# A Strassen-like product sum kept in PSUM by a ScalarE copy, and the remainder's operands made on VectorE

## What is computed

```python
# attention part: a gated recurrence over S=768 steps, B=2, H=8 heads, D=40 (run in chunks of 128 tokens)
C = f_stab * C + i_stab * outer(v_t, k_t);  n = f_stab * n + i_stab * k_t
y[:, :, t] = sigmoid(o_gate) * (C @ q_t) / maximum(abs(n . q_t), 1.0)
# mixture-of-experts part on x = y as (1536, 320), 4 experts, hidden width 1024
p = domain_probs / (domain_probs.sum(-1, keepdims=True) + 1e-09)
for e in range(4):
    h = np.maximum(x @ w1[e], 0.0)
    out += p[:, e:e + 1] * (h @ w2[e])
```

## Time and profile before

| | us |
|---|---|
| median of 3 runs (421.38 to 422.93) | 422.16 |
| the profiled execution | 421.93 |
| its span, first to last instruction | 420.2 |
| PE busy in it | 405.5 (97%) |
| DVE, POOL, ACT busy | 276.8, 209.5, 191.4 |
| PE idle before its instructions, put down to DVE's L1181 | 5.0 |

### The profile page before, as it was taken

The page is one execution under the profiler, slowest core; times in us unless marked ns, Lnnn a source line. Parts: engine busy times, 40 slices in busy tenths (PEclk is TensorE's granted clock), DMA queues, the critical chain, the costliest instruction groups (busy, mean ns, idle before and its releaser), DMA issues.

```text
span 420.2 us, 7279 instructions
## 1 busy us (share of the span) xinstructions
PE 405.5 (97%) x2650; PEld 389.8 (93%) x2650; DVE 276.8 (66%) x484; ACT 191.4 (46%) x378; POOL 209.5 (50%) x233
## 2 busy tenths in 40 slices
PE   8999999999999999999996999989999999999997
PEld 8899999998999999999995989877999999999997
DVE  5885796759545448355369862468767776787853
ACT  4575477858352657324033422524443345333420
POOL 4865734577831759604109801653555536456300
PEclk9999999999999999999999899999999999999999
DMA  8899839676860605305034001221122201230002
GB/s 266 271 289 397 350 105 357 217 250 242 278 267 0 222 2 220 123 1 211 0 67 99 0 2 68 97 81 42 41 83 81 81 10 73 83 97 18 1 2 94
DMA packets 18053, 54.49 MB, mean 130 GB/s; under 512 B 2177, under 2 KB 8850, under 8 KB 16866
## 3 DMA queue, kind: packets, MB, share of 16 engines
q1 hardware_dynamic: 17442, 52.63, 36.4%
q10 hardware_dynamic: 576, 1.40, 1.0%
HBM read 50.40 MB, written 2.05 MB: 125 GB/s over the span
## 4 chain that ended last, share of the span: by engine, by line
PE 84%; DVE 8%; issue 3%; POOL 3%; ACT 2%; DVEq 0%; ACTq 0%; POOLq 0%
PE hid_ps L1602 18%; PE acc_ps L1621 18%; PE acc_ps L1685 14%; PE out_ps L1558 4%; PE hid_ps L1685 3%; PE acc_ps L1602 2%; PE out_ps L1565 2%; PE out_ps L1661 2%; PE out_ps L1662 2%; PE out_ps L1664 2%; PE out_ps L1663 2%; PE hid_ps L1451 1%; PE score_ps L1502 1%; PE add_ps L1661 1%; PE score_ps L1661 1%
## 5 line engine op out<-in xcount | busy, mean ns | idle before, releaser
L1181 DVE SCALAR_TENSOR_TENSOR h_lo<-hid_ps,h_hi 128x384 fp32r<-128x384 f32 (+1 forms) x70 | 35.9, 513 | 89.2 <-ACT h_hi L842 88.9
L842 ACT ACTIVATE h_hi<-hid_ps 128x384 fp32r<-128x384 f32 (+1 forms) x70 | 31.9, 456 | 112.4 <-PE hid_ps L1602 112.3
L1621 PE MATMUL acc_ps<-w_hi,h_hi 128*128 128x320 f32 x208 | 66.8, 321 | 6.3 <-DVE h_lo L1181 5.0
L1621 PE MATMUL acc_ps<-w_hi,h_lo 128*128 128x320 f32 x208 | 64.5, 310 | 0.0
L1621 PE MATMUL acc_ps<-w_lo,h_hi 128*128 128x320 f32 x208 | 64.2, 309 | 0.0
L613 POOL TENSOR_TENSOR w_lo<-w_raw,w_hi 128x384 fp32r<-128x384 f32 x40 | 46.8, 1174 | 21.8 <-ACT w_hi L828 21.7
L1602 PE MATMUL hid_ps<-xt_hi,w_hi 128*128 128x384 f32 (+1 forms) x210 | 57.1, 326 | 0.1
L1602 PE MATMUL hid_ps<-xt_hi,w_lo 128*128 128x384 f32 (+1 forms) x210 | 56.6, 323 | 0.0
L1621 PEld LDWEIGHTS acc_ps<-w_hi,h_hi 128*128 128x128 f32 x208 | 39.4, 189 | 8.1 <-DVE h_lo L1181 6.4
L587 POOL TENSOR_SCALAR_AFFINE_SELECT dec_w<-dec_w 128x512 f32<-128x512 f32 x22 | 16.4, 743 | 50.3 <-ACT dec_w L807 50.3
L1621 PEld LDWEIGHTS acc_ps<-w_lo,h_hi 128*128 128x128 f32 x208 | 39.4, 189 | 0.1
(11 more groups left out here) (256 smaller groups left out, 1036.2 us busy)
## 6 DMA issues: line engine op xcount, KB each, us to landing
w_raw<-in_w_b SPq DMA_DIRECT2D x19, 704.0 KB, 7.5
w_raw<-in_w_s SPq DMA_DIRECT2D x12, 832.0 KB, 4.4
raw<-in_qk_s SPq DMA_DIRECT2D x8, 1024.0 KB
g_all<-g_dram SPq DMA_DIRECT2D x10, 512.0 KB, 7.1
kv<-in_kv_n SPq DMA_DIRECT2D x12, 352.0 KB, 6.5
q_pack<-in_q_p SPq DMA_DIRECT2D x10, 192.0 KB, 7.5
out_y<-y_acc SPq DMA_DIRECT2D x12, 160.0 KB, 1.8
carry<-g_dram SPq DMA_DIRECT2D x30, 60.0 KB
```

What stands on the lines that cost most here:

```text
L842: nc.scalar.activation(h_hi[:, M % RING, 0:cols], hid_bank(M)[:, 0:cols], ACT.Relu).then_inc(hid_hi, 1)
L1181: nc.vector.scalar_tensor_tensor(h_lo[:, M % RING, 0:cols], hid_bank(M)[:, 0:cols], 0.0, h_hi[:, M % RING, 0:cols].bitcast(fp32), ALU.max, ...
L1621: last = nc.tensor.matmul(acc_ps[t][:, 0:DM], x, w, start=(f == 0 and i == 0), stop=(f == NF - 1 and i == 2))
```

## The change

Product 1 is copied by ACT from `score_ps` into `out_ps`, and products 6, 7 and 4 accumulate on it; ACT, not DVE, then copies the sums out after product 6 (`keep_2`) and after product 7 (`keep_3`), and `add_21` falls away. The order of the products is 1, 5, 6, 7, 2, 4, 3. One matmul into `out_ps` ahead of step 0 sets that bank up for accumulation. `rest_whole` and `turn_rest` go from POOL to DVE, and the preparation is spread over slots 64 to 74; both `step_sums` on POOL come earlier; step 0's products start in slot 73. Tiles 7 to 11 have their attention, casts and subtractions one slot earlier, with an exception in each table. The loads of the first two weight steps stand in slots 54 and 55 of SP's list.

```diff
-T0 = {2: 2, 3: 6, 4: 16, 5: 22, 6: 30, 7: 35, 8: 41, 9: 47, 10: 51, 11: 57}
+T0 = {2: 2, 3: 6, 4: 16, 5: 22, 6: 30, 7: 34, 8: 40, 9: 46, 10: 50, 11: 56}
-CAST = {4: (11, 12), 5: (16, 17), 6: (24, 25), 7: (28, 31), 8: (36, 38), 9: (42, 44), 10: (45, 48), 11: (52, 53)}
-SUB = {4: (13, 14), 5: (18, 19), 6: (26, 27), 7: (32, 33), 8: (38, 40), 9: (44, 46), 10: (48, 49), 11: (54, 56)}
+CAST = {4: (11, 12), 5: (16, 17), 6: (24, 25), 7: (28, 30), 8: (35, 37), 9: (41, 43), 10: (44, 47), 11: (51, 52)}
+SUB = {4: (13, 14), 5: (18, 19), 6: (26, 27), 7: (31, 32), 8: (37, 39), 9: (43, 45), 10: (47, 48), 11: (53, 55)}
-ORDER = (1, 6, 5, 7, 2, 4, 3)
+ORDER = (1, 5, 6, 7, 2, 4, 3)
-BEGIN = 72
+BEGIN = 73
...
 # SP
-                if M == T0[NT - 1] + 4:
-                    load_step(0)
-                    load_step(1)
+                if M in (54, 55):
+                    load_step(M - 54)
...
 # POOL, slots
-                if M == 64: step_sums(0)
-                if M == 65: own_lows(0); rest_whole(0); turn_rest(1)
-                if M == 66: rest_whole(1); turn_rest(2)
-                if M == 69: step_sums(1)
-                if M == 71: own_lows(1)
+                if M in (59, 61): step_sums((M - 59) // 2)
+                if M in (65, 67): own_lows((M - 65) // 2)
...
 # ACT
-            def keep_1(t):
+            def spread_1(t):
                 act.wait_ge(product_done, product_count(t, 1))
...
-                wait_if(act, whole_of[21], t)
-                nc.scalar.activation(kept_1[:, 0:width(t)], wide_bank[1][:, 0:width(t)], ACT.Copy).then_inc(kept_1_done, 1)
+                wait_if(act, low_of[21], t)
+                nc.scalar.activation(out_ps[:, 0:width(t)], score_ps[:, 0:width(t)], ACT.Copy).then_inc(kept_1_done, 1)
+            def keep_2(t):
+                act.wait_ge(product_done, product_count(t, 6))
+                wait_if(act, whole_of[12], t)
+                nc.scalar.activation(sum_2[:, 0:width(t)], out_ps[:, 0:width(t)], ACT.Copy).then_inc(sum_2_done, 1)
+            def keep_3(t):
+                act.wait_ge(product_done, product_count(t, 7))
+                wait_if(act, whole_of[22], t)
+                nc.scalar.activation(sum_3[:, 0:width(t)], out_ps[:, 0:width(t)], ACT.Copy).then_inc(sum_3_done, 1)
...
 # ACT, slots and steps
-                if M == 79: wide_relu(0, 21); own_highs(2); sums_highs(2)
+                if M == 79: wide_relu(0, 21)
+            own_highs(2)
             wide_relu(0, 12)
+            sums_highs(2)
             wide_relu(0, 22)
             for t in range(1, STEPS):
                 if 1 < t < STEPS - 1:
                     own_highs(t + 1)
-                keep_1(t)
+                spread_1(t)
                 if 1 < t < STEPS - 1:
                     sums_highs(t + 1)
+                keep_5(t)
                 if t + 1 < STEPS:
                     step_down_high(t + 1)
-                keep_5(t)
+                keep_2(t)
+                keep_3(t)
...
 # DVE: add_2, add_3, add_21 removed; slots
+                if M == SLOTS - 1:
+                    add_expert(M // NF, (0,)); wide_low(0, 21); add_expert(M // NF, (1, 2))
+                if M == 64: make_whole(0); turn_whole(0)
+                if M == 65: make_whole(1); turn_whole(1)
+                if M == 66: turn_whole(2); turn_whole(3); sums_lows(0)
+                if M == 67: rest_whole(0); turn_rest(0)
+                if M == 68: rest_whole(1); turn_rest(1)
+                if M == 69: turn_rest(2); turn_rest(3)
+                if M == 70: rest_lows(0)
+                if M == 71: t_lows(0)
+                if M == 72: step_rest_low(0); t_lows(2)
+                if M == 73: rest_lows(1)
+                if M == 74: sums_lows(1); step_rest_low(1)
...
 # PE, in product(t, m)
                 if m == 1:
                     if t == 0:
-                        pe.wait_ge(rest_low, 2)
-                        pe.wait_ge(t_low, 2)
+                        pe.wait_ge(rest_low, 1)
                         pe.wait_ge(p_ready, 2 * NT)
+                        pe.wait_ge(xt_done, NT)
+                        nc.tensor.matmul(out_ps[:, :], left_lo[:, 0, 0, :], xt_hi[:, 0, 0:WIDE], start=True, stop=True)
+                elif m == 5:
+                    pe.wait_ge(sums_low, t + 1)
+                    if t == 0:
+                        pe.wait_ge(rest_low, 2)
+                        pe.wait_ge(t_low, 2)
+                    wait_if(pe, low_of[12], t)
                 elif m == 6:
-                    pe.wait_ge(sums_low, t + 1)
-                    wait_if(pe, low_of[21], t)
+                    pe.wait_ge(kept_1_done, t + 1)
...
-                nc.tensor.matmul(to, hi[:, 0:128], x_hi, start=m in (1, 5, 6), stop=False, skip_group_check=True)
+                nc.tensor.matmul(to, hi[:, 0:128], x_hi, start=m in (1, 5), stop=False, skip_group_check=True)
```

More of the change, by code:

```diff
@@ L743, in _ @@
                     split_low(w)
[L744 to L760, removed]
+                if M in (59, 61):
+                    step_sums((M - 59) // 2)
+                if M in (65, 67):
+                    own_lows((M - 65) // 2)
+                if M in (75, 77):
+                    step_down_low((M - 75) // 2)
+                if M == 78:
                     add_22(0)
-                if M == 78:
                     step_sums(2)
@@ L957, in _ @@
                     gate_open(first)
+                if M == 64:
+                    own_highs(0)
                 if M == 65:
[L959 removed]
                     sums_highs(0)
[L961 to L963 removed]
+                if M == 66:
+                    own_highs(1)
+                    sums_highs(1)
+                if M in (67, 68):
+                    round_t(2 * (M - 67))
                 if M == 69:
                     round_rest(0)
[L966 to L967 removed]
+                if M == 71:
                     round_rest(1)
[L969 to L972 removed]
+                if M == 74:
+                    spread_1(0)
                 if M == 75:
+                    keep_5(0)
                     step_down_high(0)
[L975 removed]
+                if M == 76:
+                    keep_2(0)
                 if M == 77:
+                    keep_3(0)
                     step_down_high(1)
@@ L1183, in hidden_low, with add_expert @@
                     .then_inc(hid_lo, 1)
-            def add_expert(at):
+            def add_expert(at, ts=(0, 1, 2)):
                 load, first_tile, tiles = GROUPS[at]
-                for t in range(tiles):
+                for t in ts[:tiles]:
                     n = first_tile + t
@@ L1358, in _ @@
                     hidden_low(ahead)
-                if M == 79:
-                    wide_low(0, 21)
-                    add_12(0)
                 if M == 0:
@@ L1382, in _ @@
                     keep_heads(k)
-                if M % NF == NF - 1:
+                if M == SLOTS - 1:
+                    add_expert(M // NF, (0,))
+                    wide_low(0, 21)
+                    add_expert(M // NF, (1, 2))
+                elif M % NF == NF - 1:
                     add_expert(M // NF)
@@ L1401, in _ @@
                 if M == 71:
+                    t_lows(0)
+                if M == 72:
+                    step_rest_low(0)
+                    t_lows(2)
+                if M == 73:
                     rest_lows(1)
-                if M == 72:
+                if M == 74:
                     sums_lows(1)
-                if M == 73:
                     step_rest_low(1)
-                if M == 74:
-                    add_2(0)
-                if M == 76:
-                    add_3(0)
                 if M == 78:
                     wide_low(0, 11)
-                    add_21(0)
+            add_12(0)
+            wide_low(0, 12)
             sums_lows(2)
             step_rest_low(2)
-            wide_low(0, 12)
             wide_low(0, 22)
@@ L1425, in _ @@
                 add_wide(t, 2)
-                add_3(t)
                 add_wide(t, 3)
                 wide_low(t, 11)
-                add_21(t)
                 wide_low(t, 21)
```

106 lines of the change are left out of this document (37 added, 69 removed).

## The result

| | before | after |
|---|---|---|
| median, us (4 runs each, side by side) | 422.55 (421.38 to 424.06) | 417.12 (416.24 to 418.35) |
| the profiled execution | 421.93 | 417.27 |
| its span | 420.2 | 415.0 |
| PE, DVE, ACT, POOL busy | 405.5, 276.8, 191.4, 209.5 | 404.0, 243.5, 205.2, 195.5 |

The ratio is 0.987, with a 95% interval of 0.983 to 0.991: the change makes the kernel 1.3% faster. 414.8 had been forecast, with a range of 412.4 to 417.8, so the time is inside the range and 2.3 us above the forecast.

What follows compares the result with a forecast made beforehand. PE was taken as the bound, losing 8.0 us from 219.64 to 247.63 because DVE was late. The terms -8.0 + 0.25 - 1.25 + 1.6 + 0.9 - 0.7 + 0.45 - 0.35 = -7.1 take 421.93 to 414.8, range 412.4 to 417.8.

Steps and rivals of the forecast that it cites:

- rival 1: Slots 64 to 73: DVE stays late, 2 to 4 us of the loss stay, 417 to 419; chance 0.17.
- Part 2: Ahead of product 1 of step 0: one more 512-column matmul on PE's path, +0.25 us.
- Part 3, slots 40 and 56: With the attention tables shifted, PE's waits for evictions at these slots (idle 0.40 each) go, -1.25 us.
- Slot 32: `SUB[7]` puts a subtraction in slot 31 ahead of evictions, delaying PE's first down here: +1.6 us, between 1.2 and 2.2.
- rival 3: Steps: `keep_2` is late in every step by 0.3 to 0.5 us, about 418.5; chance 0.08.
- Part 4: The steps: PE's work unchanged, DVE's freed time worth nothing by itself, only latencies count; +0.3 us in all.
- (a): Steps: `keep_2` delays product 7 by 0.1 us in seven later steps, plus 0.2 once in step 2; +0.9 us.
- (b): Steps 1 and 2: 3.3 us of old waits go, product 5's late operand loses 1.7 and 0.9; -0.7 us.
- (c): Step 11: product 5's operand comes late, as no down follows product 3 of step 10; +0.45 us.
- rival 2: The slot 32 stall does not come and `keep_2` is hidden, 412.5; chance 0.18.
- rival 4: Steps: ACT becomes the bound, product 7 comes 0.8 us later in 11 steps, 423.5, slower than before; chance 0.03.
- rival 5: PE's stalls around 230 us come from semaphores or loads, not DVE's queue; 8.0 us stay, 422.5; chance 0.03.

Runs made afterwards that it cites:

- experiment 5: The kernel of experiment 1 with the remainder's six operations on DVE all in slot 67 instead of 67 to 69; 416.01 us, ratio 0.982.
- experiment 4: The kernel of experiment 1 with the remainder's six operations back on POOL, spread over slots 67 to 69; 415.19 us, ratio 0.980.
- experiment 7: The kernel of experiment 1 with the old product scheme, `keep_1(1)` and `add_2(1)` placed ahead of step 2's preparation; 411.63 us, ratio 0.972.
- experiment 1: The changed kernel with tile 7's two subtractions in slots 32 and 33 instead of 31 and 32; 414.02 us, ratio 0.979.
- experiment 2: The kernel before with tile 7's subtractions moved to slots 31 and 32 and its second cast to slot 30; 425.89 us, ratio 1.007.
- experiment 6: The changed kernel with the old product scheme (SBUF copy, DVE additions, old order, no extra matmul), preparation kept; 419.7 us, ratio 0.992.
- experiment 3: The changed kernel with the tables `T0`, `CAST` and `SUB` as before the change; 415.45 us, ratio 0.983.
- experiment 8: The kernel of experiment 1 with product order 1, 5, 6, 2, 7, 3, 4 in steps 0 to 10 and some downs moved; 411.56 us, ratio 0.971.
- experiment 9: The kernel of experiment 8 with `SUB[10]` at (48, 49) and result 21 ahead of 22 in step 1; 409.86 us, ratio 0.968.

## Why the prediction was right or wrong, step by step

**What bounds the kernel before:** right. The 8.0 us lost in the earlier trace rows came back in full: from M = 65 to 79 the difference moved by 8.7, which is 8.0 less the extra matmul (0.25) and plus the product (0.95) that changed sides. No idle and full clock in 220 to 245 show it, and DVE's operations there have the lengths taken from the earlier trace rows, as in after's

```profile
227.60 1.20 DVE L1257 TENSOR_TENSOR rest_hi<-rest_hi,rest_lo 96x1024 f32<-96x1024 f32 x1
...
244.05 2.28 DVE L1284 TENSOR_TENSOR rest<-rest_lo,rest 32x2048 fp32r<-32x2048 f32 x1
```

The account of DVE's load slot by slot held; rival 1 (DVE stays late) fell. Only its slack had been set a little wide, as the 1.65 us of experiment 5 show, where 1 was expected from it. What the prediction didn't separate was the engine from the place: experiments 4 and 5.

**Part 2, the extra matmul:** +0.25, right: 0.2 by the starts of `hidden_low` in experiment 7, which doesn't have it, against experiment 1.

**Part 3, slots 40 and 56:** right, 0.6 each. **Slot 32: this is the step that failed, by its size.** The prediction named the mechanism, the place and the queue, and gave +1.6, within 1.2 to 2.2, from the subtraction's old place beside POOL. It was 3.3. The idle grew by 2.2, the prediction's upper bound and for its reason, POOL's low part going first (the rows of slot 31 above). At full clock that stall costs 1.9 (experiment 2), inside the bounds; 1.4 came on top at half clock. The sum had left out the clock, though the prediction read in the earlier trace rows that a long idle stood right ahead of half clock there. **The second miss is "behind that slot no other wait is tight":** slot 48 has a wait of 0.33 for the same reason (`SUB[10]` now has a subtraction in slot 47, ahead of the evictions), 0.4 us. The reasoning that worked for slot 31 had not been put to every slot with M = 7 modulo 8. The two misses, 1.7 and 0.4, are the distance between -7.1 and the -5.2 by the spans (0.2 went the other way, ahead of slot 32). So the measured 417.12 lies above the 413.6 to 416.2 that were given to the forecast itself, and inside the stated range only by the part that was kept for rivals 1 and 3, which both fell: the range was right by its width.

**Part 4:** right in its sum (+0.3 predicted, +0.3 measured), but two of its terms are off and cancel, which is luck. (a) Of `keep_2`: 0.1 a step was predicted. In step 3 of after, product 6 takes 0.93 us up to the next down (295.38 to 296.31), product 7 takes 1.00 (297.19 to 298.19), so 0.07, and the step as a whole takes 13.61 instead of 13.53. Over seven steps that is 0.6, where the sum had 0.9. ACT's copy (296.51 + 0.60) ended 0.08 us ahead of product 7:

```profile
295.38 0.39 PE L1643 MATMUL out_ps<-t_hi,left_hi 128*128 128x512 f32 x1
...
296.31 0.46 PE L1667 MATMUL acc_ps<-w_hi,w_lo 128*128 128x320 f32 x2
...
297.19 0.47 PE L1643 MATMUL out_ps<-t_hi,left_hi 128*128 128x512 f32 x1
...
298.19 0.46 PE L1667 MATMUL hid_ps<-w_hi,w_lo 128*128 128x320 f32 x2
...
296.51 0.60 ACT L867 ACTIVATE sum<-out_ps 128x512 f32<-128x512 f32 x1 [0.58 <-PE out_ps L1646]
```

The 0.2 more for a backlog of ACT in step 2 did not show (product 6 started at 281.77, product 7 at 283.58, the plain 1.81). (b) Product 5 of step 1 lost 1.48 + 0.15, against 1.7, and that of step 2 0.73 + 0.16, against 0.9. (c) Step 11: 0.45 by the starts, as predicted. At the end of the steps 0.35 were to go, with the wait for `add_21`. It went, but a wait for DVE's evictions came in its place, the 0.15 at 406.68 above, which the sum did not have: from product 3 of step 11 to the last down it is 8.95 us before and 8.86 after, so 0.1 went. Rivals 2 to 5 fell: slot 32 did stall, `keep_2` was late by less than 0.1, ACT is no bound at 49%, and the stalls around 230 us were DVE's queue.

What the prediction did not ask was what Part 4 is for. It gave the steps +0.3 against the kernel before, but not against the old scheme behind the new preparation, which is the version to beat: there the scheme costs 2.4 (experiment 7). Of the old scheme's stalls in steps 1 and 2, those of 0.53 and 1.12 us are gone in experiment 7, those of 0.34 and 0.39 stay.

The Trainium skill has the rule that was drawn on for the SBUF lock (SBUF, State Buffer; section "SBUF: two separate sides"). The traces go on agreeing: in experiment 4 an operation of 0.68 alone took 2.88 beside POOL's 2.85 and ended 0.54 us behind it (224.29 + 2.88 against 223.78 + 2.85), and slot 31's subtraction, 1.2 alone, took 2.05 behind POOL's 0.99. By that rule the term for slot 32 should have been the upper bound, 1.2 + 0.99 = 2.2, and not the nearest row.
The Trainium skill also says that PSUM is ScalarE's faster destination (ScalarE: Activation LUTs, section "Step-by-step: what each stage is for"), which no row could bear out before. Here the copy of 512 columns out of PSUM took 0.58 to 0.59 us into PSUM (8 copies) and 0.60 into SBUF (16 copies), so the difference is 0.02 us at most. One of each in after:

```profile
246.83 0.59 ACT L861 ACTIVATE out_ps<-score_ps 128x512 f32<-128x512 f32 x1
...
282.90 0.60 ACT L867 ACTIVATE sum<-out_ps 128x512 f32<-128x512 f32 x1
```

## What to carry to other kernels

When one engine is near full and its stalls come from another's queue, price every operation that is put ahead of what it waits for, in every slot of that kind and not only in the one that stands out, and bound it by everything that can hold it up in turn. A change with two halves should be measured in halves: here one (the preparation, spread and moved) brought more than the whole, and the other gave some of it back until its order was changed. And a stall can cost more than its idle: a long one may be followed by half clock, in one execution and not in the next.

## What the runs showed of the hardware that was not expected

- The same idle of 2.79 to 2.80 us before the down of slot 32 was followed by 3.4 us of half clock in after, by 6.8 us in experiment 6 and by none in experiment 2, where a half clock stretch stood at 278 to 282 behind idles of 1.12 and 0.53 instead, idles behind which the kernel before ran at full clock. In these traces every half clock stretch in the midst of the work stood behind idle time of PE, but how long the idle is doesn't tell whether one comes. What decides it stays open. In the profiled executions of the versions whose longest stall is 1.65 us or less (experiments 1, 3, 4, 5, 7, 8, 9) there is none, and the mean granted clock of the span is 0.999 or 1.000 in all their 30 runs.
- It changes from one execution to the next of the same kernel. One stretch of 3.4 us brings the mean granted clock of the span to 0.996 (the profiled executions of before and after), two bring it to 0.992 (experiment 2), 10.2 us in all to 0.988 (experiment 6). Of after's four runs three have 0.996 and the fastest, 416.24 us, has 1.000; of the 28 runs of before beside the experiments three have 1.000, seven 0.996, seventeen 0.992 and one 0.988. So the half clock of slot 32 was in most runs of after and not in all, and no figure for it holds for a kernel in general.
- ScalarE's copy from PSUM to PSUM takes nearly as long as from PSUM to SBUF (0.58 to 0.59 and 0.60 for 128 x 512).
- Between VectorE and GpSimd it is not only VectorE that is held up: in slot 31 of after POOL's low part of 128 x 320 took 1.84 us beside the subtraction, where the same one took 0.88 at this place in the kernel before.
